# Attention stage of a one-core kernel: scores and transposes taken in groups of two tiles, PSUM banks tied to engines, and one load put behind another

## What is computed

```
scores = q @ k^T / 8 + cum[i] - cum[j]      (causal; cum = running sum of log f)
attn   = softmax(scores);  x = attn @ v      (4 x 8 heads, 576 tokens, 64 wide)
x      = rms_norm(x) * gain                  (2304 tokens, 512 wide)
x      = (silu(x @ w_gate) * (x @ w_val)) @ w_out
out    = silu(x @ w_in) @ w_out2
```

## Time and profile before

| | us |
|---|---|
| median of three runs | 987.19 |
| lowest, highest | 986.37, 988.20 |
| the profiled execution, whole | 987.51 |
| its span in the trace | 985.8 |
| PE busy in the span | 978.8 (99%) |
| DVE, ACT, POOL busy | 643.9, 454.6, 342.3 |

### The profile page before, as it was taken

How to read it: one execution, slowest core, us unless ns; L and a number is a source line. 1 busy time by engine, 2 the same in 40 slices (tenths; PEclk the granted TensorE clock), 3 DMA queues, 4 the chain that set the end, 5 groups by cost and what they waited for, 6 DMA issues and landing times.

```text
span 985.8 us, 16401 instructions
## 1 busy us (share of the span) xinstructions
PE 978.8 (99%) x5807; PEld 889.8 (90%) x5807; DVE 643.9 (65%) x1265; ACT 454.6 (46%) x975; POOL 342.3 (35%) x318
## 2 busy tenths in 40 slices
PE   8999999999999999999999999999999999999998
PEld 5777776899999999999999999989989899898996
DVE  6777789688758797788682787704837148371441
ACT  6877787545254235245242343523615236152341
POOL 6777755603302563235334243120221202212022
PEclk9999999999999999999999999999999999999999
DMA  7667565276826666569479477342563425634212
GB/s 200 209 189 240 157 186 160 97 288 232 302 108 258 265 223 228 200 258 346 160 277 338 187 258 270 125 171 90 192 256 117 168 100 189 254 113 171 107 34 95
DMA packets 74144, 192.68 MB, mean 195 GB/s; under 512 B 8464, under 2 KB 38928, under 8 KB 67920
## 3 DMA queue, kind: packets, MB, share of 16 engines
q1 hardware_dynamic: 74064, 191.64, 54.6%
HBM read 150.12 MB, written 41.49 MB: 194 GB/s over the span
## 4 chain that ended last, share of the span: by engine, by line
PE 94%; DVE 3%; ACT 1%; DMA 1%; issue 1%; SPq 0%; POOL 0%; ACTq 0%; DVEq 0%; POOLq 0%
PE banks L1878 19%; PE banks L1880 19%; PE banks L1879 19%; PE banks L2011 7%; PE banks L2010 7%; PE banks L2009 7%; PE banks L1768 5%; PE banks L1804 5%; PE banks L1720 4%; PE banks L1780 1%; DMA cum_b<-cum_dram 1%; DVE wu L1396 0%; DVE scratch L1567 0%; PE banks L1733 0%; DMA cum_dram<-zeros 0%
## 5 line engine op out<-in xcount | busy, mean ns | idle before, releaser
L1878 PE MATMUL banks<-xb,wu 128*128 128x384 f32 x864 | 289.0, 334 | 0.0
L1880 PE MATMUL banks<-xb,wu 128*128 128x384 f32 x864 | 288.7, 334 | 0.0
L1879 PE MATMUL banks<-xb,wu 128*128 128x384 f32 x864 | 288.6, 334 | 0.0
L856 POOL TENSOR_TENSOR wd<-stage_d,wd 128x512 fp32r<-128x512 f32 x84 | 118.2, 1413 | 470.2 <-ACT wd L1057 470.2
L1878 PEld LDWEIGHTS banks<-xb,wu 128*128 128x128 f32 x864 | 162.2, 188 | 0.4 <-issue 0.2
L1879 PEld LDWEIGHTS banks<-xb,wu 128*128 128x128 f32 x864 | 162.2, 188 | 0.2
L1880 PEld LDWEIGHTS banks<-xb,wu 128*128 128x128 f32 x864 | 162.2, 188 | 0.0
L1139 ACT ACTIVATE scratch<-scratch 128x384 f32<-128x384 f32 x144 | 75.3, 523 | 113.0 <-DVE scratch L1525 51.2
L1148 ACT ACTIVATE hid_main<-scratch 128x384 fp32r<-128x384 f32 x144 | 72.2, 517 | 117.8 <-DVE scratch L1567 117.8
L1057 ACT ACTIVATE wd<-stage_d 128x512 fp32r<-128x512 f32 x84 | 51.6, 629 | 138.2 <-PE banks L2011 100.3
L1574 DVE TENSOR_TENSOR hid_main<-scratch,hid_main 128x384 fp32r<-128x384 f32 x144 | 88.3, 627 | 40.6 <-ACT hid_main L1148 36.3
(11 more groups left out here) (190 smaller groups left out, 1718.3 us busy)
## 6 DMA issues: line engine op xcount, KB each, us to landing
wu<-kept SPq DMA_DIRECT2D x48, 1792.0 KB, 9.9
stage_d<-w SPq DMA_DIRECT2D x84, 256.0 KB, 2.8
kept<-ws SPq DMA_DIRECT2D x14, 1024.0 KB, 5.3
kept<-wu SPq DMA_DIRECT2D x12, 768.0 KB, 4.5
qk_raw<-qk_t SPq DMA_DIRECT2D x14, 576.0 KB, 3.4
cum_b<-cum_dram SPq DMA_DIRECT2D x30, 256.0 KB, 4.3
kept<-xb SPq DMA_DIRECT2D x6, 1024.0 KB, 5.3
kept<-ws SPq DMA_DIRECT2D x8, 768.0 KB, 5.1
```

The source lines that it names most:

```text
L856: nc.gpsimd.tensor_tensor(wd[:, d % 2, 1, :], stage_d[:, d % 2, :], f32(wd[:, d % 2, 0, :]), ALU.subtract).then_inc(wd_split, 1)
L1878: nc.tensor.matmul(dst, w_hi_part, m_hi, start=start, stop=False)
L1879: nc.tensor.matmul(dst, w_hi_part, m_lo, start=False, stop=False)
L1880: return nc.tensor.matmul(dst, w_lo_part, m_hi, start=False, stop=stop)
```

## The change

Nothing of what is computed changes. On PE the groups S0 and S1 now run one after the other, as do S2 and S3. The turn's order is: S0, S1; both(p-1,2); S2, S3; both(p-1,3); values part 0 of p-1; t0 and t1 of p-1; S4; row_factors(p-1); values part 1 of p-1, all five blocks; both(p,1); and a new entry-less step, `first_transposes(p)`, which turns tiles 0 and 1 into the free half of bank 6 in one go. DVE copies both out with one instruction (`take_first`). Entries on an even place are all copied by ACT and those on an odd one by DVE, so bank 4 is always ACT's and bank 5 DVE's. The mean is made in two halves of 192 columns, one after both(p-1,2) and one after both(p-1,3). The orders of ACT and DVE are rewritten to fit. SP waits until the running sums of pair 1 have landed before it issues q and k of pair 2.

```diff
-ORDER = (0, 1, "r0", "r1", 2, 3, 4, 5, 6, 7, "t0", "t1")
-BY_ACT = frozenset((1, 3, 4, 6, "t0", "r0"))
+ORDER = ((4, 1), (5, 1), (6, 1), (7, 1), ("t0", 1), ("t1", 1), ("r0", 1), ("r1", 1), (2, 0), (3, 0))
+BY_ACT = frozenset((2, 4, 6, "t0", "r0"))
...
             load_cum(1)
+            sp.wait_ge(cum_in[1], 48)
             load_qk(2)
             load_v(0)
```

ACT's order after:

```
...
+            exps(0, 3)
             for p in range(NPAIRS + 1):
+                here = p < NPAIRS
+                if 0 < p < NPAIRS:
+                    exps(p, 0)
+                    exps(p, 1)
+                if p > 0:
+                    take_out(p - 1, 4)
+                if 0 < p < NPAIRS:
+                    exps(p, 2)
+                    exps(p, 3)
+                if p == GUESS_PAIR + 1:
+                    guess_exp(0)
+                if p == NPAIRS:
+                    xb_high(0, "B12")
+                if p > 0:
+                    take_out(p - 1, 6)
+                    take_out(p - 1, "t0")
+                if here:
+                    exps(p, 4)
+                    exps(p, 5)
...
+                    exps(p, 6)
...
+                if p > 0:
+                    row_scales(p - 1)
+                if p == NPAIRS - 1:
+                    xb_high(0, "B11")
+                if here:
+                    exps(p, 7)
+                    exps(p, 8)
                 if p == PREP_PAIR:
                     w_raw(0)
                 if p == PREP_PAIR + 1:
                     w_raw(1)
+                if p == GUESS_PAIR:
+                    guess_log(0)
                 if p == NPAIRS - 1:
                     xb_high(0, "B21")
+                if 0 < p < NPAIRS:
+                    take_out(p, 2)
```

```diff
+                if p > 0:
+                    x_out(p - 1, 0)
                 if p == GUESS_PAIR + 1:
                     newton_step(0, 0, 0)
                     newton_step(0, 0, 1)
                 if p == GUESS_PAIR + 2:
+                    newton_step(0, 1, 0)
                     newton_step(0, 1, 1)
                     newton_step(0, 2, 0)
                 if p == GUESS_PAIR + 3:
+                    newton_step(0, 2, 1)
                     normalise_x(0, 0, 0)
                     normalise_x(0, 1, 0)
+                if p == GUESS_PAIR + 4:
+                    normalise_x(0, 2, 0)
+                    normalise_x(0, 3, 0)
+                    normalise_x(0, 0, 1)
                 if p > 0:
+                    x_out(p - 1, 1)
+                if p == GUESS_PAIR + 4:
                     normalise_x(0, 1, 1)
```

PE's new steps and order:

```diff
+            def first_transposes(p):
+                pe.wait_ge(exped, TILES * p + 2)
+                if p > 0:
+                    wait(pe, x_done, 2 * (p - 1) + 1)
...
+                for s in range(2):
+                    last = nc.tensor.transpose(first_turn_view[:, P * s:P * (s + 1)], probs[s][:, 0:P], ident[:, :])
+                last.then_inc(first_turned, 1)
...
             for p in range(1, NPAIRS):
                 scores(p, 0)
                 scores(p, 1)
+                both(p - 1, 2)
+                if p in MEAN_PAIRS:
+                    first_mean(MEAN_PAIRS.index(p), 0)
                 scores(p, 2)
+                scores(p, 3)
+                both(p - 1, 3)
+                if p in MEAN_PAIRS:
+                    first_mean(MEAN_PAIRS.index(p), 1)
+                values(p - 1, 0, (0, 1))
+                last_tile(p - 1)
+                scores(p, 4)
+                row_factors(p - 1)
...
+                values(p - 1, 1, range(NT))
+                both(p, 1)
+                first_transposes(p)
...
             both(NPAIRS - 1, 2)
             pe.wait_ge(shifted, TILES * (NPAIRS - 1) + TAIL)
             plain_product(0, 0, 0)
+            both(NPAIRS - 1, 3)
             values(NPAIRS - 1, 0, (0, 1))
+            last_tile(NPAIRS - 1)
             pe.wait_ge(shifted, TILES * NPAIRS)
             plain_product(0, 0, 1)
             row_factors(NPAIRS - 1)
+            values(NPAIRS - 1, 1, range(NT))
```

More of the change, by code:

```diff
@@ L1427, in _ @@
                                     ALU.subtract).then_inc(qk_split, 1)
+            shift(0, 3)
             for p in range(NPAIRS + 1):
-                here, following = p < NPAIRS, p + 1 < NPAIRS
+                here = p < NPAIRS
+                if p > 0:
+                    take_out(p - 1, 3)
+                    take_first(p - 1)
+                if 0 < p < NPAIRS:
+                    for r in range(4):
+                        shift(p, r)
+                if p > 0:
+                    take_out(p - 1, 5)
+                if p in MEAN_PAIRS:
+                    take_first_mean(MEAN_PAIRS.index(p), 0)
                 if here:
-                    shift(p, 3)
+                    shift(p, 4)
+                    shift(p, 5)
+                    shift(p, 6)
                 if p > 0:
                     take_out(p - 1, 7)
-                if p > 1:
-                    x_out(p - 2, 1)
-                if p == GUESS_PAIR + 2:
-                    newton_step(0, 1, 0)
-                if p == GUESS_PAIR + 3:
-                    newton_step(0, 2, 1)
-                if p == GUESS_PAIR + 4:
-                    normalise_x(0, 2, 0)
+                if p in MEAN_PAIRS:
+                    take_first_mean(MEAN_PAIRS.index(p), 1)
+                if p > 0:
+                    invert(p - 1)
+                if here:
+                    shift(p, 7)
+                if p > 0:
+                    take_out(p - 1, "t1")
+                if 0 < p < NPAIRS - 1:
+                    qk_round(p + 1)
                 if p == NPAIRS:
@@ L1627, in plain_cycle @@
                         w_sums(q)
-            x_out(NPAIRS - 1, 1)
             for g in range(NHALF):
@@ L1795, in values @@
                     pe.wait_ge(out_dve, copies(ready, False))
+                    if part == 0:
+                        pe.wait_ge(out_first, p + 1)
                     wait(pe, x_done, 2 * (p - 1) + part + 1)
@@ L1837, in both, with last_tile @@
                 transposes(p, 2 * i + 1, 2 * i + 1, range(i + 1))
+            def last_tile(p):
+                transposes(p, TAIL, "t0", range(NFULL))
+                transposes(p, TAIL, "t1", range(NFULL, NT))
             scores(0, 0)
@@ L1842, in _ @@
             scores(0, 2)
+            scores(0, 3)
             pe.wait_ge(cum_taken, 4)
-            both(0, 0)
-            scores(0, 3)
             both(0, 1)
```

159 lines of the change are left out of this document (44 added, 115 removed).

## The result

The changed kernel took 1003.35 us (median of 4 executions, 1001.44 to 1003.99), the kernel before beside it 986.78: a ratio of 1.0163, interval 1.0151 to 1.0175. It is slower, as forecast, but by 16.6 us instead of 4.8, and outside the range. The profiled execution of the changed kernel was its fastest, 1001.44 us with a span of 999.7; the span before was 985.8, so the two traces have to account for 13.9 us. All of it is there when the dense stage begins (188.40 before, 202.33 after); from there on both run alike.

What follows compares the result with a forecast made beforehand. The prediction took PE's own list of matmuls, plus any waits the new order puts on PE, as the bound. Its terms, -7.7 + 5.0 + 1.2 + 0.7 + 1.8 + 2.4 + 1.4 = +4.8, gave 992.0 us, range 988.0 to 996.5.

Steps and rivals of the forecast that it cites:

- Margin 0.05: Plain turn: the spread of the factors ends at 6.42, 0.05 us before PE needs it; taken as met.
- term 1: Turns 2 to 14: fewer switches on PE shorten each turn from 10.70 to 10.11, -7.7 us.
- Rival (c): Factors' chain misses its margin by 0.1 to 0.2 a turn, values land at 23: 994 to 997 us; chance 0.22.
- The low parts: Plain turn: POOL's low parts end at 9.8, before the next S0 at 10.11; taken as met.
- Rival (e): PE's clock falls to its lower level behind the mean's waits and the one for values, adding 7: 999 us; chance 0.04.
- Term 2: Turns 9 and 10: PE waits 2.3 us before S2 for the mean's sums, +5.0 us in all.
- Term 3: Turn 1: values of pair 0, issued later, are there at 21.0, so S0 of turn 2 starts later, +1.2 us.
- Term 4: ACT's extra work ahead of its copy of entry 2: +0.7 us over turns 3 and 4, +1.8 for turn 12.
- Terms 5 and 6: Newton steps and normalisations delaying DVE's copies and shifts, +2.4 us; waits in the tail before the dense product, +1.4 us.

Runs made afterwards that it cites:

- e3: Changed kernel with the scaling (rest_scale) made by DVE behind the reciprocal instead of by POOL behind the spread; 1009.39 us, ratio 1.0225.
- e5: Changed kernel with one added wait: DVE's cast of the next q and k starts only after POOL's scaling; 1008.55 us, ratio 1.0214.
- e9: Changed kernel with the mean's halves later, no SP wait, cast behind the scaling, DVE's steps spread, half the cast on ACT; 987.19 us, ratio 0.9999.
- e10: Changed kernel with only the cast's wait on the scaling and half of the cast moved to ACT; 1001.66 us, ratio 1.0155.
- e1: Changed kernel with 30 unneeded matmuls on PE before the mean's first half in turns 9 and 10; 999.95 us, ratio 1.0129.
- e4: Changed kernel without SP's wait for the running sums of pair 1 ahead of the third pair's q and k; 1000.72 us, ratio 1.0138.
- e7: Changed kernel with DVE's Newton steps and normalisations of turns 12 to 15 spread over its idle places; 996.32 us, ratio 1.0093.

## Why the prediction was wrong

**The step that failed: "Margin 0.05 ... I take both as met" in term 1.** The walk of the factors ended at the spread, taken at the 1.08 of the earlier trace rows. It put POOL's scaling behind it, 0.44 in the kernel before, at nothing, and did not ask what made the spread take 1.08. The cast did. In the new order the reciprocal came later than walked (the spread started 5.51 after S0, where the walk had the reciprocal done at 5.27), the spread took 0.61 and was done at 6.12 for 6.42, so the margin that was doubted held, by luck. The cast fell on the scaling instead, which took 1.09 and was done at 7.19, and PE stood for it in twelve turns. Rival (c) had the factors' chain late by 0.1 to 0.2 a turn, at 0.22; it was 0.38.

The low parts, put at a margin of 0.3, were closer as well: they started 7.15 after S0 instead of 6.87 and ended at 10.07, against a turn of 10.24 without waits. e3 and e5, which both move the cast back, made S0 wait for them. That the scaling could be had at 0.44 without moving the cast is not shown by any run; e9 and e10 had to halve the cast.

**The size of the merge was also off, by less.** Without waits the turn is 10.24 (e9, e10), so the new order saves 0.46, where 0.59 was worked out. By the distances in e10's turn 6 and in the earlier trace rows the two merged blocks of scores saved 0.17 and 0.20 (0.22 each was taken) and the merged transposes 0.07 (0.13); the factors with the product behind them cost 0.10 more where 0.03 less was taken; and t0 and t1 saved 0.10 that was not forecast. Of the 6.7 us by which term 1 failed, 13 x 0.13 = 1.7 are this, and 13 x 0.38 = 4.9 the wait.

**Rival (e), given 0.04, happened.** It said that the clock would fall behind the waits at the mean and for v, up to 7 us. In the profiled execution it fell behind one of the means, where the rival had it, and in the tail, where it did not, for 3.5 us in all; in the others it cost about 5, by their mean clocks. e1 shows the cause for the means. The reason given against it, that holes of up to 1 us had left the clock at 1.00, says nothing of holes of 2 us and more, and the prediction itself forecast four of these.

**Term 2 was right**: PE waits 2.0 (2.3 forecast), the two turns cost 4.4 without the clock (5.0). **Term 3 was right**: v comes into use at 21.4 (21.0), +1.5 for +1.2, and e4 confirms it. The figure of the Trainium skill that the prediction sets beside it (DMA: Bandwidth & Descriptors, Anatomy of one DMA), under 3 us to land, is fitted on that page to DMAs that GpSimd issues. SyncE issues these, and v came into use 5.9 us after its issue. **Term 4 was too dear**: w_raw cost nothing in turns 3 and 4, presumably because the turn was 0.5 longer than forecast and ACT had that slack; turn 12 was 1.3 longer than a plain turn, where turn 11 before was 0.33 longer, so +1.0 for 1.8. **Terms 5 and 6 were right in their sum but for the clock**, 4.2 for 3.8, and right in that DVE's steps were to blame, as e7 bears out. In the turns PE stood one step before S2, where the prediction had it: at the transposes of tile 5, for DVE's copy of entry 3 (the fifth wait in the list above, the longest 0.7). And in the tail the steps were priced at 0.73 each, with no term for the one that took 2.17 beside POOL, so part of that agreement is luck.

The sum again: 4.8 + 6.7 (term 1) + 3.5 (clock) - 1.2 (the other terms) = 13.8, against 13.9 in the spans. The direction rested on terms 2 to 6, which held in their sum; the size on the one term that was a gain.

## What to carry to other kernels

A chain that is met by 0.05 us is a coin toss: follow it to its last operation, and before an order is changed ask, for each duration used, what ran beside it, since a collision between DVE and POOL moves along with the order. Price a wait of 2 us or more on TensorE with the clock behind it. And a reordering that shortens a dense turn by a few per cent is worth having only when everything placed around the turn (loads, means, table loads, steps for the next stage) is fitted anew to it: here that fitting was worth 15 us, the reordering itself at most 6 (13 turns of 0.46), and no version measured was faster than the kernel before.

## What the runs showed of the hardware

- The clock fell behind waits of 2.0 to 2.8 us, but not each time: behind the wait of 2.02 in turn 9 it stayed at 1.00 in the profiled execution of the changed kernel, and in e4_nosp it fell at the same place. In e9_best it was low from 19.3 to 22.7 after waits of 1.12 and 0.34 us close together, with none of 2 us near.
- DVE's cast of 1280 fp32 columns from SBUF to SBUF, running beside an operation of POOL, lengthens it: 0.61 to 1.08 (spread), 0.44 to 1.09 (scaling), while DVE's shift out of PSUM beside the spread does not (0.61). The other way round, POOL's subtraction of 768 columns lengthened one of DVE's normalisations from 0.61 to 2.17.
- The 320 KB of v came into use 4.9 to 6.3 us after its issue in seven kernels with the same loads in the same order (19.75 to 21.48), a spread that turn 1 passes on.
